# Attention on one core: a group's products with the values in two pieces instead of three

## The reference, cut to what matters

```python
# q, k, v: 2 batches, 8 heads, 768 rows, 64 columns; proj: 64 x 6; all float32
q_bucket, k_bucket = bits_to_number(q @ proj > 0), bits_to_number(k @ proj > 0)
scores = (q @ k.T) / 8
scores = where(q_bucket[:, None] == k_bucket[None, :], scores, -1e9)
attn = exp(scores - max(scores)); attn = attn / (sum(attn) + 1e-9)
x = attn @ v                       # per head, then heads side by side: 1536 x 512
x = moe(x)                         # 8 experts, capacity 192
out = moe2(x)                      # skip gate, 8 experts
```

## Time and profile before

| | |
|---|---|
| median of 3 runs | 642.27 us (640.92 to 644.3) |
| profiled execution: span, first to last instruction | 638.8 us |
| profiled execution: its own time | not given apart from the span, which is 2.1 below the lowest run |
| TensorE: matrix products busy | 620.4 us, 97% |
| TensorE: weight loads busy | 484.4 us, 76% |
| VectorE busy | 360.6 us, 56% |
| ScalarE busy | 295.1 us, 46% |
| POOL busy | 146.8 us, 23% |
| attention | up to about 253 us of the span |

### The profile page before, as it was taken

How to read it: one execution, slowest core, us unless ns; L and a number is a source line. 1 busy time by engine, 2 the same in 40 slices (tenths; PEclk the granted TensorE clock), 3 DMA queues, 4 the chain that set the end, 5 groups by cost and what they waited for, 6 DMA issues and landing times.

```text
span 638.8 us, 11468 instructions
## 1 busy us (share of the span) xinstructions
PE 620.4 (97%) x4384; PEld 484.4 (76%) x4384; DVE 360.6 (56%) x1132; ACT 295.1 (46%) x525; POOL 146.8 (23%) x152
## 2 busy tenths in 40 slices
PE   6999999999999999888999999999999999999997
PEld 3777776777677766367898989898999877777773
DVE  6876777677777776886868778786522220000000
ACT  5867777777776767542525343452212111111111
POOL 5340303031222911210100101010333123333201
PEclk9999999999999999989999999999999999999999
DMA  8947936455464100371634435373798769999970
GB/s 191 235 91 160 216 81 155 108 125 125 109 194 95 47 10 1 113 274 42 249 124 166 157 133 179 135 249 102 271 345 313 268 223 330 353 341 353 335 271 20
DMA packets 73394, 116.38 MB, mean 182 GB/s; under 512 B 33800, under 2 KB 37162, under 8 KB 73059
## 3 DMA queue, kind: packets, MB, share of 16 engines
q1 hardware_dynamic: 68738, 106.75, 54.6%
q0 software_dynamic: 4016, 8.80, 4.0%
q10 hardware_dynamic: 576, 0.01, 0.0%
HBM read 87.76 MB, written 12.23 MB: 157 GB/s over the span
## 4 chain that ended last, share of the span: by engine, by line
PE 87%; issue 6%; DVE 3%; DMA 1%; ACT 1%; POOL 1%; SPq 0%; POOLq 0%; DVEq 0%
PE psB L1061 12%; PE psB L1075 12%; PE psB L353 10%; PE psB L338 9%; PE psB L1807 9%; PE psB L1822 9%; PE psA L323 7%; PE psA L325 5%; PE psB L368 2%; PE psA L997 1%; PE psB L281 1%; PE psB L1098 1%; PE psB L292 1%; PE psB L1992 1%; PE psB L1047 1%
## 5 line engine op out<-in xcount | busy, mean ns | idle before, releaser
L474 DVE TENSOR_REDUCE mx<-psA 128x1 f32<-128x768 f32 x96 | 91.8, 956 | 52.0 <-PE psA L325 50.6
L542 ACT ACTIVATE prob<-psA,ebi,esc 128x768 f32<-128x768 f32 x96 | 95.2, 992 | 23.9 <-DVE ebi L419 19.5
L1061 PE MATMUL psB<-xgT,w 128*128 128x192 f32 x512 | 93.3, 335 | 0.4 <-ACT xgT L1161 0.3
L1061 PEld LDWEIGHTS psB<-xgT,w 128*128 128x128 f32 x512 | 84.2, 193 | 7.1 <-issue 3.8
L1075 PE MATMUL psB<-hT,w 128*128 128x192 f32 x512 | 88.2, 329 | 0.0
L1075 PEld LDWEIGHTS psB<-hT,w 128*128 128x128 f32 x512 | 82.7, 190 | 0.3
L338 PE MATMUL psB<-cst,prob 128*128 128x128 f32 x576 | 78.8, 273 | 0.3
L323 PE MATMUL psA<-kH,qT 128*128 128x384 f32 x192 | 74.2, 387 | 2.8 <-ACT kB L581 1.6
L338 PEld LDWEIGHTS psB<-cst,prob 128*128 128x128 f32 x576 | 66.8, 140 | 5.3 <-DVE pT L487 1.9
L353 PE MATMUL psB<-pT,v_in 128*64 128x384 f32 x360 | 68.0, 499 | 0.0
L593 ACT COPY pT<-psB 128x512 f32<-128x512 f32 x96 | 55.9, 582 | 25.4 <-PE psB L338 24.6
(11 more groups left out here) (289 smaller groups left out, 874.6 us busy)
## 6 DMA issues: line engine op xcount, KB each, us to landing
w<-in_moe_w SPq DMA_DIRECT2D x34, 2048.0 KB
kH<-hi SPq DMA_DIRECT2D x30, 192.0 KB
q_in<-in_q SPq DMA_DIRECT2D x16, 192.0 KB, 3.9
k_in<-in_k SPq DMA_DIRECT2D x16, 192.0 KB, 4.3
v_in<-in_v SPq DMA_DIRECT2D x8, 384.0 KB, 3.4
x_scratch<-x_of_batch SPq DMA_DIRECT2D x2, 1536.0 KB, 6.5
x_scratch<-x SPq DMA_DIRECT2D x8, 384.0 KB
qT<-hi SPq DMA_DIRECT2D x15, 192.0 KB
```

Of the source, the lines that this page charges most:

```text
L474: nc.vector.tensor_reduce(mx[:, u:u + 1], psS[u % 2][:, :, 0:HALF], AX.XY, ALU.max).then_inc(s_dv, 1)
L542: nc.scalar.activation(prob[:, u % 2, :, :], psS[u % 2][:, :, 0:HALF], ACT.Exp, bias=ebi[:, u:u + 1], scale=esc[:, u:u + 1], accum_out=den ...
L1061: ins = nc.tensor.matmul(ps[:, (f % 2) * CAP:(f % 2 + 1) * CAP], w1[:, k % 2, d, f * P:(f + 1) * P], xgT[:, k % 2, d, :], start=d == 0, st ...
```

## The change

A group's products with the values are made in two pieces of three key blocks, after tiles 1 and 4, instead of three pieces of two, after tiles 1, 3 and 5. The turned pieces (prep 0 to 3), which came at tiles 2 and 4, come at tiles 2 and 3. The signs piece, which came behind the PV piece of tile 5 (once, in group 0, at tile 1), comes behind that of tile 4 (in group 0 still at tile 1). In group 15 the two pieces follow tiles 1 and 3. The copy of `xun` is tied to the last piece of `PVC` and moves with it. The whole diff:

```diff
@@ plan()
-        if G < NGRP - 1 and n in (2, 4) and todo and todo[0][2] < 4:
+        if G < NGRP - 1 and n in (2, 3) and todo and todo[0][2] < 4:
             steps.append(todo.pop(0))
         steps.append(("T", u))
         if G == NGRP - 1:
-            steps.append([("X", G - 2), ("PV", G - 1, 0), ("PV", G - 1, 1), ("PV", G - 1, 2), ("X", G - 1), None][n])
-            if n == per - 1:
-                steps.pop()
+            steps += [[("X", G - 2)], [("PV", G - 1, 0)], [], [("PV", G - 1, 1)], [("X", G - 1)], []][n]
             continue
-        if G and n % 2:
-            steps.append(("PV", G - 1, n // 2))
+        if G and n in PIECE_AT:
+            steps.append(("PV", G - 1, PIECE_AT.index(n)))
         if G > 1 and n == 0:
             steps.append(("X", G - 2))
         elif G == ROWS_AT and n and n % 2 == 0:
             steps.append(("rows", n // 2 - 1))
-        elif todo and todo[0][2] == 4 and n % 2:
+        elif todo and todo[0][2] == 4 and n in PIECE_AT:
             steps.append(todo.pop(0))
     assert not todo
     return steps + [("end", 0), ("more", ), ("end", 1), ("end", 2), ("X", NGRP - 1)]

-PVC = [[0, 1], [2, 3], [4, 5]]
+PVC = [[0, 1, 2], [3, 4, 5]]
+
+PIECE_AT = (1, 4)
```

## The result

The kernel after takes 647.85 us (median of 6 runs, 645.86 to 649.28) against 642.37 (6 runs, 640.92 to 644.3): a ratio of 1.0083, 95% interval 1.0057 to 1.0109. It is slower by 5.5 us, where 4.3 were forecast. The profiled execution took 645.86 us with a span of 643.9, so some 2.0 us lie around the span.

A forecast was written before the change was run, and what follows sets the result against it. TensorE bounds the kernel, with a 3.77 us floor per two neighbouring tiles from the exponential loop. Group terms +0.1, 0, +3.0, +0.6, +0.9, -0.3 total +4.3, on 642.27 giving 646.6 us; range 643.0 to 650.0.

The forecast's parts named there:

- Step 1: PV pieces of each group: two of 2.25 us replace three of 1.61, so products take 4.50 instead of 4.83, 0.33 less.
- Step 2: Tiles 5 and 0 of neighbouring groups: 3.49 us of TensorE work against a 3.77 floor, 0.28 wait in each of 14 transitions.
- the smaller wait hidden within: Tile 0 behind bare tile 5: wait for VectorE's copy of turned probabilities, 0.23 us, not added since 3.49 + 0.23 is under 3.77.
- Step 3: Tiles 2 and 3: wait before tile 4's scores, 0.35 us in groups 1 to 11, 0.68 in 12, 1.01 in 13 and 14.
- Step 4: ScalarE's two turned-piece copies in neighbouring tiles: second exponential 0.1 us late, costing nothing in groups 1 to 12, 0.1 in group 0.
- Step 5: The xun copy and odd groups' signs product move a tile earlier, and SP and POOL queues keep their order: no cost.
- Step 6: Group 15: saves 0.33 us, pays 0.28 and 0.23, and X's wait for xun shrinks by 0.46; sum -0.3.
- TensorE alone: Rival: the 3.77 floor belongs to group 0 only and only switches count, 5.0 us less, 637.3; chance 0.07.
- A smaller loss: Rival: floor 0.1 to 0.3 us lower in middle groups, both waits shrink, 642.7 without any at tiles 2 and 3; chance 0.31.
- A long piece that saves nothing: Rival: a three-block PV piece takes 2.42 us, so the 5.0 saving goes, 651.6; or late exponentials pile up; chance 0.06.
- The clock: Rival: the granted clock falls in the new waits; given no chance of its own, as it reads 1.00 in group 0.
- The carry-over to the end: After attention everything hangs on its end, so the +4.3 us is carried to the kernel's end one for one.

The follow-up runs named there:

- second profiles: Both kernels profiled again without edit; groups 1 to 15 (first scores of group 1 to end of attention) take 227.10 us after against 221.86 before.
- experiment 5: Kernel before with six PV pieces of one key block, one after each tile (group 15: two after each of three); groups 1 to 15 take 238.56 us, +16.7.
- experiment 7: Kernel after with TensorE's wait for placed operands one tile earlier for pairs 2 to 7; groups 1 to 15 take 226.72 us, 0.4 less.
- experiments 2 and 3: Twelve turned pieces done twice: groups 1 to 15 227.16 us (after), 225.60 (before). Kernel after, scale and bias ahead of VectorE's copy at tile 2: 225.10.
- experiment 6: Kernel after with the signs piece of odd groups behind tile 5 instead of tile 4; groups 1 to 15 take 226.50 us, 0.6 less.
- swap2: Label not defined in the text; perhaps the kernel after with scale and bias ahead of VectorE's copy at tile 2, groups 1 to 15 225.10 us.
- before_double: Kernel before with the turned piece of tile 4 done twice for pairs 2 to 7; groups 1 to 15 go from 221.86 to 225.60 us.
- after_double: Kernel after with the turned piece of tile 3 done twice for pairs 2 to 7; groups 1 to 15 take 227.16 us, 0.06 more.

## Why the prediction was right, point by point

The mechanism came out as forecast; the size is a fifth short. The sum from group 1 on was 4.2 (4.3 less the 0.1 of group 0), and 5.25 was measured between the second profiles. By parts:

| part | forecast | measured |
|---|---|---|
| group 1 | 0 | +0.14 |
| groups 2 to 11 | +3.0 | +3.8 (even +0.36, odd +0.41 each) |
| group 12 | +0.6 | +0.6 |
| groups 13 and 14 | +0.9 | +0.9 |
| group 15 | -0.3 | -0.3 |

Step 1, fewer pieces: a piece of three blocks takes 2.26 (2.25 foreseen), and a group's products 4.52 against 4.83. Its fixed part is confirmed by the straight line of experiment 5. By the rule of the Trainium skill (TensorEngine Tiling, Tiling Modes) that a change of tiling mode drains TensorE, each switch saved is a gain; the trace agrees, with 0.32 per piece, though no run separates a drain from other costs of a switch. (The weight-load idles of 0.17 and 0.60 in the forecast mark the place of this cost and not its size.) As a forecast of the change the rule fails, since it speaks only of TensorE.

Step 2, tiles 5 and 0: 0.29 per transition, 0.28 foreseen. The sign named for it, idle time of 0.28 on the scores that ScalarE's exponential ends, isn't in the profile: what shows is 0.35 ahead of the transposes, for the copy that the forecast called the smaller wait hidden within. Step 3, tiles 2 and 3: 0.36 in even groups against 0.35. There the sign shows. What was too small is its term for odd groups and group 13: 0.45 there, since the scores of tile 4's step carry two waits in them, and the second instruction shows as soon as TensorE is not ahead of its work. Since tile 4 is 0.03 shorter for it, this costs 0.06, and seven times 0.06 is 0.4 of the 1.0 us that the sum lacked; experiment 7 moves six of the seven waits and gets 0.4 back. Before the change it cost nothing: tile 3 takes 2.98 or 2.99 in even and odd groups alike. The other 0.6 is some 0.06 in each of groups 1 to 11, by differences of 0.01 to 0.02 in these three terms and in the lengths before (14.47 or 14.48 in even groups, where the forecast's prices add up to 14.50).

Step 4: the second copy on ScalarE makes the exponential of tile 3 0.11 late (2.75 after its scores instead of 2.64) and nobody waits for it. The 0.1 for group 0 can't be seen, since group 0 moves by 1.4 us from run to run. Step 5, moved copies and signs: nothing waits for them in groups 2 to 12 that the waits list doesn't name. Step 6, group 15: -0.3, and X comes 0.74 behind its transposes (252.81 to 253.55 in the second profile after) instead of 1.24.

Rivals. TensorE alone: falls with experiments 2 and 3. A smaller loss: the floor in the middle groups is 3.78, not below that of group 0, though group 0 moves more than twice the bytes per microsecond. A long piece that saves nothing: falls with experiment 5. The clock: 1.00 in groups 6 and 13 after, with the waits.

The carry-over to the end held, but is only seen within some 2 us, since the rest of the program varies by more.

## What to carry to other kernels

On a busy in-order engine, work of other kinds between two uses of a double buffer is cover for the chain that frees it. Count it pair by pair, not on average: here an average group had 14.2 us of TensorE work against six times 1.88, and still two pairs fell short. Merging pieces to save a switch (0.32 us) takes cover away at two places, and here cost twice what it saved: 0.29 + 0.36 a group against 0.31. Where the sum of a pair falls below the chain's length, an added instruction is free and a removed one gains nothing.

## What the runs showed of the hardware that was not expected

A second semaphore wait ahead of an instruction, satisfied long before, costs 0.09 us where TensorE is stalled there, of which the next tile gets 0.03 back; moved to a place where TensorE doesn't wait, it costs nothing that can be seen (experiment 7). What makes the 0.09 was not tried.

The cost of narrow weights hangs on what stands before: the signs piece, eight instructions with 32-column weights, takes 0.78 behind products with 64-column weights and 0.96 behind full-width transposes (experiment 6; the 0.78 is also there in the kernel before, 3.77 less 2.99 at tile 5).

What follows attention took 387.2 to 393.9 us with the same instructions, and the granted clock goes with it. In the first profile of before it reads 0.50 from 281 to 284 us, which is the lower level, 1.2 GHz instead of 2.4, and 1.00 again after 285. The first 16 products of L1061, which lie there, take 4.52 us; in the second profile of before, where the clock stays at 1.00, they take 2.84. Five of the thirteen profiled executions have such a stretch between attention and the last microsecond (before, the second one of after, swap2 and before_double one, after_double two), and they took 389.0 to 393.9 us there; the other eight took 387.2 to 388.7. Ahead of each such stretch TensorE had been idle for between 1.46 and 2.18 us, waiting for a DMA. But the second profile of before has 1.49 us of the same wait and before_double 2.30, and there the clock doesn't fall. What decides that stays open; no run was made for it.
